# Retention followed by two expert layers on one core: decay tables made on TensorE, and another order of the first loads and of the folded quarters

## The reference

```
scores = q @ k^T / sqrt(64)                 # 8 batches, 8 heads, 576 positions, head size 64
gamma  = 1 - 2 ** (-5 - h)                  # one per head h
D[i,j] = gamma ** (i - j) if i >= j else 0
x      = (scores * D) @ v                   # -> 4608 x 512
h      = max(x @ w1, x @ w2, x @ w3)        # 512 -> 768
y      = h @ w_out                          # 768 -> 512
z      = ((y @ u1) * (y @ u2)) @ u3 @ u_out # 512 -> 1024 -> 1024 -> 512
```

## Time and profile before

| | us |
|---|---|
| median of 3 runs (lowest, highest) | 1234.87 (1234.5, 1235.02) |
| the profiled execution, its own time | 1234.69 |
| its span in the profile | 1232.9 |
| PE busy in the span | 1216.6 (99%) |
| DVE, ACT, POOL busy | 761.3, 486.4, 433.7 |
| retention, first to last of its PE work | 4.42 to 177.47 |

### The profile page before, as it was taken

One profiled execution on the slowest core, in us unless ns is written; L12 is line 12 of the kernel. 1 busy time (PEld: TensorE's weight loads), 2 busy tenths in 40 slices (PEclk: granted clock), 3 DMA queues, 4 the chain that ended last, 5 costly groups with the idle time before them and its releaser, 6 DMA issues. The chain is left out here.

```text
span 1232.9 us, 21160 instructions
## 1 busy us (share of the span) xinstructions
PE 1216.6 (99%) x8288; PEld 1202.2 (98%) x8288; DVE 761.3 (62%) x1192; ACT 486.4 (39%) x779; POOL 433.7 (35%) x234
## 2 busy tenths in 40 slices
PE   6999999999999999999999999999999999999999
PEld 5999999999999999999999999999999999999998
DVE  5666957844546364658876777453535366776553
ACT  3433544523223232326555544242323234554441
POOL 2644628220100102052967761202020217366550
PEclk9999999999999999999999999999999999999999
DMA  9999944120202112053455441213131343444441
GB/s 332 322 335 352 337 144 163 46 84 33 96 27 88 41 52 77 27 173 127 170 208 195 156 154 59 103 52 109 52 116 52 110 165 109 154 154 161 156 159 65
DMA packets 88084, 169.96 MB, mean 138 GB/s; under 512 B 9904, under 2 KB 59184, under 8 KB 87984
## 3 DMA queue, kind: packets, MB, share of 16 engines
q1 hardware_dynamic: 87984, 168.60, 39.3%
HBM read 106.70 MB, written 61.87 MB: 137 GB/s over the span
## 5 line engine op out<-in xcount | busy, mean ns | idle before, releaser
L1100 PE MATMUL ps<-chi,whi 128*128 128x384 f32 x2016 | 674.2, 334 | 2.1 <-ACT w L831 1.1
L1102 PE MATMUL ps<-chi,wlo 128*128 128x384 f32 x2016 | 673.5, 334 | 0.0
L1101 PE MATMUL ps<-clo,whi 128*128 128x384 f32 x2016 | 673.5, 334 | 0.0
L589 POOL TENSOR_TENSOR raw<-raw,raw 128x768 f32<-128x768 f32 (+3 forms) x102 | 267.1, 2640 | 588.8 <-DMA raw<-xd 203.6
L1100 PEld LDWEIGHTS ps<-chi,whi 128*128 128x128 f32 x2016 | 378.4, 188 | 4.2 <-ACT w L831 1.8
L1101 PEld LDWEIGHTS ps<-clo,whi 128*128 128x128 f32 x2016 | 378.5, 188 | 0.0
L1102 PEld LDWEIGHTS ps<-chi,wlo 128*128 128x128 f32 x2016 | 378.5, 188 | 0.0
L840 DVE TENSOR_TENSOR clo<-raw,chi 128x768 fp32r<-128x768 f32 (+2 forms) x168 | 252.4, 1530 | 31.8 <-ACT chi L763 31.8
L763 ACT CAST chi<-raw 128x768 fp32r<-128x768 f32 (+2 forms) x168 | 180.4, 1081 | 85.4 <-PE ps L1102 53.4
L831 ACT COPY w<-ps 128x384 f32<-128x384 f32 x126 | 60.6, 481 | 240.7 <-PE ps L1102 239.2
L818 ACT COPY u<-ps 128x384 f32<-128x384 f32 x126 | 60.7, 481 | 160.6 <-PE ps L1102 158.9
(11 more groups left out here) (43 smaller groups left out, 829.9 us busy)
## 6 DMA issues: line engine op xcount, KB each, us to landing
qks<-qk SPq DMA_DIRECT2D x32, 576.0 KB, 7.0
gd<-h SPq DMA_DIRECT2D x96, 192.0 KB, 1.9
raw<-gd SPq DMA_DIRECT2D x24, 768.0 KB, 6.0
hd<-h SPq DMA_DIRECT2D x72, 192.0 KB, 1.9
raw<-hd SPq DMA_DIRECT2D x24, 576.0 KB, 5.8
x2d<-h SPq DMA_DIRECT2D x48, 192.0 KB, 2.5
raw<-x2d SPq DMA_DIRECT2D x24, 384.0 KB, 4.6
outT<-h SPq DMA_DIRECT2D x48, 192.0 KB, 1.9
```

Of the source, the lines that this page charges most:

```text
L589: return nc.gpsimd.tensor_tensor(out_, a, b, op)
L1100: nc.tensor.matmul(to, w1, x1, start=(start and k == 0), stop=False, skip_group_check=True)
L1101: nc.tensor.matmul(to, w1, x2, start=False, stop=False, skip_group_check=True)
L1102: last = nc.tensor.matmul(to, w2, x1, start=False, stop=(k == KH[st] - 1), skip_group_check=True)
```

## The change

- The tables are no longer loaded. A small array `pows` (8 x 896) is loaded instead, and PE makes outer products of powers: `decay_powers(i)` (two matmuls of 256 columns) for `dec`, `query_powers` (one of 512 columns) for `qtab`. DVE multiplies the first by a causal mask (`mask_decay`, two instructions of 128x512) into `dec`; ACT copies the second into `qtab`. `cols` (128 x 140) holds `vtab`, a column table that is not used, and the mask.
- PE runs matmuls on a zeroed tile `idle` whose results are thrown away: five at its start, three more at each of three places around the second pair's scores and state. ACT copies one column of `idle` first.
- The first two pairs have key buffers of their own (`ks_first`), so the keys of pairs 2 and 3 are loaded at the start, and `load_k` waits only from pair 4 on. In steps 1 to 3 the keys are issued first in a step. From pair 4 on the values of two pairs come in one DMA, and the tails have DMAs and semaphores of their own.
- `uo` is loaded one part in step 1 and three in step 2 (before two and two). Part 0 is split on DVE at the end of step 2, part 1 on POOL in step 3, parts 2 and 3 on POOL in step 4.
- Quarters: step 3 runs quarter 0 alone (before 0 and 1); step 4 runs quarter 1 after the scores, and quarters 2 and 3 at its end, after `values` (before 2 and 3 after the scores).
- In stages C and O each block of a tile waits for its own buffer, and in O the last block is issued ahead of one store.
- The states and all else of the retention are as they were.

Core of the diff:

```diff
 def quarters(m):
+    if m == WC_FROM:
+        return range(1)
+    if m == WC_FROM + 1:
+        return range(1, 2)
     if m >= STEPS - 2:
...
+def late_quarters(m):
+    return range(2, 4) if m == WC_FROM + 1 else ()
...
-UO_LOAD = {1: (0, 1), 2: (2, 3)}
-UO_SPLIT = {2: (0, 1), 3: (2, 3)}
+UO_SPLIT = {2: (0,), 3: (1,), 4: (2, 3)}
...
             def load_k(n):
-                if n >= 2:
+                if n >= 4:
                     sp.wait_ge(state_summed, n - 1)
-                sp.dma_start(ks[n % 2][:, :], kk[n, :, :]).then_inc(k_loaded[n % 2], 16)
+                sp.dma_start(keys_of(n)[:, :], kk[n, :, :]).then_inc(k_loaded[n % 4], 16)
...
-                    sp.wait_ge(c_lo, 7 * (tau - 1) + 4)
-                for pos in (0, 3, 6, 2):
-                    if pos != 6 or t == 0 or st != O:
-                        load_raw_block(tau, pos)
+                for pos in blocks:
+                    if t and st in (C, O):
+                        if pos != 6 or st == O:
+                            sp.wait_ge(c_lo, 7 * (tau - 1) + pos + 1)
+                    load_raw_block(tau, pos)
...
+            sp.dma_start(pows[:, :], powers).then_inc(pows_loaded, 16)
+            sp.dma_start(cols[:, :], columns).then_inc(cols_loaded, 16)
             load_qk(0)
-            load_decay(0, slice(0, 2))
-            sp.dma_start(vtab[:, :], vdecay).then_inc(vtab_loaded, 16)
             load_v(0)
             load_k(0)
             load_qk(1)
-            load_decay(1, slice(2, 4))
             load_v(1)
             load_k(1)
             load_qk(2)
-            sp.dma_start(qtab[:, :, :], qdecay).then_inc(qtab_loaded, 16)
             load_qk(3)
-            load_decay(2, slice(4, HEADS))
             load_v(2)
             load_v(3)
+            load_k(2)
+            load_k(3)
+            load_tails(0)
...
@@ ACT @@
+            act.wait_ge(idle_zeroed, 1)
+            nc.scalar.copy(idle[:, CH + 1:CH + 2], idle[:, CH:CH + 1])
+            decay_values(0)
+            act.wait_ge(qtab_powers, 1)
+            nc.scalar.copy(qtab[:, :], ps[:, S_WC, :]).then_inc(qtab_made, 1)
+            decay_values(1)
...
@@ DVE @@
+            def mask_decay(i):
+                if i == 0:
+                    dve.wait_ge(cols_loaded, 16)
+                dve.wait_ge(dec_powers, i + 1)
+                nc.vector.tensor_tensor(
+                    dec[:, i, :, :, :].rearrange("p h n c -> p (h n) c"),
+                    ps[:, 2 + i, :].rearrange("p (n c) -> p n c", c=CH),
+                    mask.unsqueeze(1).broadcast_to([P, 4, CH]), ALU.mult).then_inc(dec_made, 1)
...
                 for n in made_in(m):
                     decay_scores(n)
                     if n == 0:
+                        mask_decay(1)
                         make_state(n)
...
+                if m == 2:
+                    split_uo(0)
...
@@ PE @@
+            pe.wait_ge(idle_zeroed, 1)
+            run_idle(5, S_STATE)
+            pe.wait_ge(pows_loaded, 16)
+            decay_powers(0)
             pe.wait_ge(zeroed, 12)
             for m in range(STEPS):
                 for n in made_in(m):
                     scores(n)
-                    if m == 0:
-                        sum_state(n)
+                    if n == 0:
+                        decay_powers(1)
+                        query_powers()
+                        sum_state(0)
+                        pe.wait_ge(qtab_made, 1)
+                        run_idle(3, S_WC)
+                    if n == 1:
+                        pe.wait_ge(state_made, 2 * NC)
+                        run_idle(3, S_STATE)
+                        sum_state(1)
+                        run_idle(3, S_STATE)
                 for i in quarters(m):
                     wc_quarter(i)
...
                 for n in read_in(m):
                     values(n)
+                for i in late_quarters(m):
+                    wc_quarter(i)
```

More of the change, by code:

```diff
@@ L319, in build @@
         o += 2 * NC * P * 4
+        idle = at("idle", [P, CH + 2], f32, 21504 + 8192)
         assert o <= 150528
@@ L524, in _ @@
                         store_x(n)
-                for n in made_in(m + 2):
-                    load_v(n)
+                if m == 0:
+                    load_tails(1)
+                if 2 * m + 4 < NP:
+                    load_two_v(m + 2)
+                    load_tails(m + 2)
                 if m in WC_READ:
@@ L771, in _ @@
                     split_uo(i)
+                if m in U3_SPLIT and m != 2:
+                    split_u3(U3_SPLIT[m])
                 if m in WC_READ:
@@ L852, in decay_scores @@
                         ps[:, 2 * (n % 2) + h, :].rearrange("p (n c) -> p n c", c=CH),
-                        dec[:, 2 * p + h, :].unsqueeze(1).broadcast_to([P, NC, CH]), ALU.mult).then_inc(decayed, 1)
+                        dec[:, p // 2, h, p % 2, :].unsqueeze(1).broadcast_to([P, NC, CH]), ALU.mult
+                    ).then_inc(decayed, 1)
             def decay_tail(n):
@@ L860, in decay_tail @@
                     ps[TAIL:P, S_TAIL[0]:S_TAIL[1] + 1, (n % 2) * TAIL:(n % 2 + 1) * TAIL],
-                    dec[TAIL:P, 2 * p:2 * p + 2, TAIL:CH], ALU.mult).then_inc(decayed, 1)
+                    dec[TAIL:P, p // 2, :, p % 2, TAIL:CH], ALU.mult).then_inc(decayed, 1)
             def make_state(n):
@@ L889, in split_tokens @@
                 low(clo[st][pos][:, :, :], raw_block(tau, pos)[:, :, :], chi[st][pos][:, :, :]).then_inc(c_lo, 1)
+            nc.vector.memset(idle[:, :], 0.0).then_inc(idle_zeroed, 1)
             for i in range(4):
@@ L1047, in values @@
                         own = slice(h * DH, h * DH + DH)
-                        last = nc.tensor.matmul(ps[own, bank, cols], vs[n % 6][:, c * P + h * DH:c * P + h * DH + DH],
+                        last = nc.tensor.matmul(ps[own, bank, cols], vs[:, n % 6, c * P + h * DH:c * P + h * DH + DH],
                                                 probs[n % 4][:, h, c * CH:min(SEQ, (c + 1) * CH)],
@@ L1070, in wc_quarter, with run_idle, decay_powers, query_powers @@
                     last.then_inc(wc_done, 1)
+            def run_idle(count, bank):
+                for _ in range(count):
+                    nc.tensor.matmul(ps[:, bank, 0:CH], idle[:, 0:CH], idle[:, 0:CH], start=True, stop=True,
+                                     skip_group_check=True)
+            def decay_powers(i):
+                for h in range(2):
+                    last = nc.tensor.matmul(ps[:, 2 + i, h * 2 * CH:(h + 1) * 2 * CH], pows[:, h * P:(h + 1) * P],
+                                            pows[:, 3 * P + i * 2 * CH:3 * P + (i + 1) * 2 * CH],
+                                            start=True, stop=True, skip_group_check=True)
+                last.then_inc(dec_powers, 1)
+            def query_powers():
+                nc.tensor.matmul(ps[:, S_WC, :], pows[:, 2 * P:3 * P], pows[:, 3 * P:], start=True, stop=True,
+                                 skip_group_check=True).then_inc(qtab_powers, 1)
+            pe.wait_ge(idle_zeroed, 1)
+            run_idle(5, S_STATE)
+            pe.wait_ge(pows_loaded, 16)
+            decay_powers(0)
             pe.wait_ge(zeroed, 12)
```

144 lines of the change are left out of this document (92 added, 52 removed).

## The result

| | before | after |
|---|---|---|
| median, us (lowest to highest, runs) | 1234.94 (1234.35 to 1237.62, 8) | 1239.75 (1238.43 to 1242.36, 8) |
| the profiled execution, its own time | 1234.69 | 1238.96 |
| its span | 1232.9 | 1237.1 |
| PE busy in the span | 1216.6 | 1227.9 |

The ratio is 1.0041, with an interval from 1.0031 to 1.005: slower by about 5 us, where 1235.3 with a range of 1232.8 to 1237.3 was forecast. Rival 2, the slow pace that stays, is what happened.

The account below looks back on a forecast made before the run. The prediction took PE, busy 1216.6 us of a 1232.9 us span, as the bound. Its terms, -1.0 - 1.3 + 1.3 + 1.6 = +0.6 us on the profiled 1234.69, gave 1235.3, range 1232.8 to 1237.3.

Parts of the forecast that it names:

- Rival 2: PE's start keeps the slow pace: up to +3.8 us instead of -1.0, 1240.1 at worst; chance 0.14.
- the start: 0 to 18 us: pair 1's scores end earlier, so the chain to pair 0's query starts sooner; -1.0 us.
- keys: Step 2, state sums at 29.63 and 30.98: earlier key loads remove PE's gaps; -1.3 us (0 to 1.3).
- steps 3 to 5: Quarter 0 waits for DVE's split, a quarter is owed: +1.3 us; pair 10's scores wait for ACT: +1.6.
- the rest: Values two pairs per DMA and finer waits in C and O: 0, between -0.5 and +0.5 us.
- The bound: Upper bound of the start: slow pace throughout puts the end of pair 1's scores at 16.6, +3.8 us.
- point of decision: In the head: Rival 2 decides if pair 1's scores end later than 14.7 us.
- Tables not loaded: Table loads in the head: about 2 us less DMA time, bringing PE nothing by itself.
- rival 3: Between 34 and 44 us DMA becomes the bound, waits of 1 to 2 us: 1236.6; chance 0.18 with another rival.
- the copies' term: Steps 4 and 5: ACT copies the block before x, so PE waits before pair 10's scores; +1.6 us.

Follow-up runs that it names:

- e2: Changed kernel with the decay tables loaded from HBM as before, idle matmuls kept: 1235.24 us, ratio 0.9998.
- e11: Changed kernel with tables loaded and, in place of the table products, thrown-away stand-in matmuls over 128 rows: 1235.26 us, ratio 1.0006.
- e12: Same as e11, but the stand-in matmuls run over 8 of the 128 rows: 1238.67 us, ratio 1.0033.
- e17: Changed kernel with zeros in rows 8 to 127 of `pows`, so the table products run over 128 rows: 1234.92 us, ratio 1.0008.
- e8: Kernel before with only the two more key buffers and the keys' new places in the load order: 1235.91 us, ratio 1.0005.
- e6: Changed kernel with x of pairs 6 and 7 copied by ACT ahead of the folded block in step 4: 1237.63 us, ratio 1.0025.
- e7: Kernel before with only the changed loads of raw blocks in stages C and O (finer waits): 1232.53 us, ratio 0.9982.
- e18: Kernel before with the finer waits and idle matmuls, seven at the start and three at each of three places: 1232.93 us, ratio 0.9988.
- e19: Kernel before with the idle matmuls alone, seven at the start: 1233.81 us, ratio 0.9998.
- e13: Same as e8, but in step 2 the keys are issued behind the two parts of `uo`: 1235.87 us, ratio 1.0009.
- e5: Changed kernel with quarters and splits of before, `uo` parts 2 and 3 issued in step 2 behind keys and queries: 1246.71 us, ratio 1.0097.
- e10: Same as e5, with the tables loaded from HBM: 1241.28 us, ratio 1.0061.
- e3: Changed kernel with tables loaded from HBM and without idle matmuls: 1235.62 us, ratio 0.9997.
- e4: Changed kernel with the idle tile filled with ones instead of zeros: 1239.34 us, ratio 1.0033.

## Why the prediction was wrong

| term | forecast | profile of after | shown by |
|---|---|---|---|
| the start | -1.0 (-1.7 to +3.8) | +4.25 | e2, e11, e12, e17 |
| keys | -1.3 | -1.38 | the markers; e8 |
| steps 3 to 5 | +1.3 + 1.6 | +3.10 | the markers; e6 for the copies |
| the rest | 0 (-0.5 to +0.5) | -1.8 | e7: -2.4 in the medians |
| sum | +0.6 | +4.2 | |

**The start: the step that failed.** The forecast costed the tables at "1.1 fast, 2.0 slow" and took the fast pace from the first pair on, because "now it is busy from 1.0 us on almost without a gap". The first half holds: slow, four rows took 2.07. The second failed: PE was busy without a gap and the pace did not rise, since the products that filled the gap run over 8 rows. The bound said that pair 1's scores would then end at 16.6; they ended at 16.8, and the chain behind them took 22.34 - 16.8 = 5.5 against 5.3. So the mechanism and price of rival 2 were there, and its chance of 0.14 was the error. (Its point of decision was off by one: by the forecast's own sum the upper end of the range, 1237.3, is reached when pair 1's scores end near 13.8, not 14.7.) It rested on counting busy time and not asking what kind. The Trainium skill, TensorE: Matmul & The Clock Gate, part 1, speaks of activity that releases the throttle; I read every busy row as activity, and e11 against e12 shows that here products over 8 of 128 rows did not do what products over 128 did. With full rows (e17) the start gives -0.8 us in the profile, near the -1.0 of the forecast.

The other half of what that page says, that the moment differs from run to run, is seen in e18 against e19, two kernels with one head. It does not explain the result: the ratios of after [1.0031, 1.005] and e17 [0.9999, 1.0017] lie apart, and so do those of e12 and e11, which were measured together. It does touch the size: the +4.25 is counted from one execution of before with an early query at 18.09, and from e7's 18.68 it would be 3.7.

**Tables not loaded: right.** The profile shows no wait of PE on DMA between 30 and 60 us, as forecast. Making the tables gains nothing by itself either: padded (e17) and loaded (e2) lie at 1234.92 and 1235.24, with ratios of 1.0008 and 0.9998 whose intervals overlap.

**Keys: the number was hit in the profile, and partly by luck.** One piece of sums, -1.38. But the gap of 1.3 us is that of one execution of the kernel before: e18, e19 and e7, whose keys are loaded as before, show 0.3 us of it or none. And put into the kernel before, the same edit gives nothing (e8, e13), because ACT, or the queries and keys, are then late; the late queries and keys are rival 3's mechanism. What the keys' new places are worth in the medians of the changed kernel no run shows.

**Steps 3 to 5: right.** In step 3 a wait on DVE of 1.08 (forecast about 1.3, from a split of 1.5 us that took 1.23) and about 0.3 beside it take the place of the quarter that is not done: pair 6's and pair 8's scores are 10.11 us apart in both profiles. In step 4 the owed quarter of 1.36, the wait on ACT of 1.37 (forecast 1.6) and about 0.4 in small pieces that I don't divide make the 3.10, where 1.3 + 1.6 = 2.9 was forecast. e6 shows the copies' term alone: 1.4 in the markers from pair 8's scores on, 2.1 in the medians. Of the DVE wait and the owed quarter the profile alone speaks, because e5 and e10 lost their time elsewhere.

**The rest: the kind right, the size wrong.** The forecast set the finer waits at -0.5 to +0.5, since none of PE's waits lay in the middle of C or O. They lay at the borders, 1.1 + 0.6 + 0.4 = 2.1 us, and I did not follow them back to the raw loads. e7 gives -2.4 in the medians and -1.6 between the two profiled spans, with 1.4 of border waits gone; how the loads reach the borders step by step I have not traced. That the whole misses by 4.4 us and not by 6 is owed to this gain, which was not foreseen.

**Open.** When exactly the pace rises in a given execution was not settled; nor were other row counts of a filler than 8 and 128 tried (the scores, over 64 rows, are part of every head). Each kernel has one profile, and the tallies above are of single executions.

## What to carry to other kernels

Do not count on a filler or a helper product over few rows of the array to bring the fast pace: over 8 rows it did not here, over 128 it did. Try a thin operand padded with zeros; it cost no time here and won 4 to 5 us. And count what it adds on PE: the added rows at the fast pace (e17) and the slow pace without them (e3) cost nothing that can be measured; both together made the loss. Where an engine works in order, put what releases the bottleneck ahead of what merely became ready (2.1 us), and if a load is moved forward, look at who holds the issuing engine behind it. The one part of this change that gained clear of noise when tried alone was the plainest, the loads of raw blocks that wait for their own buffers (e7, 1232.5), so time such parts apart before you judge a bundle. A gap in one profile may be missing in the next execution of the same kernel (keys): look at a second profile before you price it.

## What was not expected of the hardware

- Over 8 rows of the array, sixteen trace rows of 128 columns took 3.77 us and the pace stayed low; over 128 rows they took 2.05 us. Ones in place of zeros in the idle tile made no difference in the changed kernel (e4).
- The granted clock read 1.00 in the first 20 us of after while the same sixteen rows took 2.08 us there and 1.16 later. It did show 0.66 in e5 when the pace fell back behind a wait of 7.67 us. The duration of a row that repeats is the better witness.
- The pace can fall again in the head: fast at 4.5, slow at 7.8 in e19.
- A DVE subtraction of 128x1536 took 4.22 us when it started 0.07 or 0.16 us after POOL's sums (e10, e2), and 1.75 when it started 0.07 us or more before them (after, e17, before).
